# Attention stage of a fused kernel: k's turns and copy ahead of y's, squares behind, a second mask that waits for the decay, an earlier signal for constants

## The reference

```python
B, H, S, D = q.shape                       # 4, 8, 768, 48
f = 1.0 / (1.0 + np.exp(-f_logit))
for t in range(S):
    state = f[:, :, t, :, None] * state + np.einsum('bhd,bhe->bhde', k[:, :, t], v[:, :, t])
    y[:, :, t] = np.einsum('bhd,bhde->bhe', q[:, :, t], state)
```

```python
h = np.maximum(x[mask] @ w1[e], 0.0)
out[mask] = gate_w[mask, None] * (h @ w2[e])
```

## Time and profile before

| | us |
|---|---|
| median of three runs | 681.18 |
| lowest, highest | 680.19, 682.83 |
| the profiled execution: whole | 683.31 |
| the profiled execution: span of the trace | 681.5 |
| TensorE busy in the span | 627.3 (92%) |
| VectorE busy | 442.8 (65%) |
| ScalarE busy | 310.7 (46%) |
| GpSimd busy | 171.2 (25%) |
| mean granted clock of TensorE | 0.969 of full speed |

### The profile page before, as it was taken

How to read it: one execution, slowest core, us unless ns; L and a number is a source line. 1 busy time by engine, 2 the same in 40 slices (tenths; PEclk the granted TensorE clock), 3 DMA queues, 4 the chain that set the end, 5 groups by cost and what they waited for, 6 DMA issues and landing times.

```text
span 681.5 us, 15527 instructions
## 1 busy us (share of the span) xinstructions
PE 627.3 (92%) x4935; PEld 587.0 (86%) x4936; DVE 442.8 (65%) x964; ACT 310.7 (46%) x519; POOL 171.2 (25%) x200
## 2 busy tenths in 40 slices
PE   4999999999639999999999999995799999999997
PEld 3778788787539999999999999894799999999997
DVE  5878998989745674948383756645267446547752
ACT  2566757766404344534343344341356336336640
POOL 7212226263440005041313224052110110110111
PEclk9999999999959999999999999997799999999999
DMA  9997887772143452718070736421385474474610
GB/s 152 138 187 154 200 128 173 109 165 47 46 151 116 160 188 102 260 34 272 23 261 32 269 103 209 164 90 63 98 281 161 145 260 133 148 254 141 235 36 24
DMA packets 144217, 100.68 MB, mean 148 GB/s; under 512 B 106319, under 2 KB 135098, under 8 KB 144176
## 3 DMA queue, kind: packets, MB, share of 16 engines
q1 hardware_dynamic: 137008, 87.42, 47.8%
q0 software_dynamic: 7168, 12.73, 5.2%
HBM read 79.46 MB, written 30.08 MB: 161 GB/s over the span
## 4 chain that ended last, share of the span: by engine, by line
PE 76%; DVE 10%; issue 6%; ACT 4%; POOL 2%; SPq 1%; DMA 0%; DVEq 0%; ACTq 0%; POOLq 0%
PE bank_a L963 7%; PE bank_a L965 7%; PE bank_a L964 7%; PE banks_y L974 3%; PE banks_y L973 3%; PE banks_y L972 3%; PE bank_b L963 3%; PE banks_s L811 2%; PE bank_b L965 2%; PE bank_b L964 2%; PE banks_s L985 2%; PE bank_b L761 2%; PE bank_b L973 2%; PE bank_b L974 2%; PE bank_b L972 2%
## 5 line engine op out<-in xcount | busy, mean ns | idle before, releaser
L1371 DVE TENSOR_TENSOR w_lo<-raw_w,w_hi 128x768 fp32r<-128x768 f32 x128 | 115.0, 951 | 34.1 <-ACT w_hi L1105 34.0
L1105 ACT ACTIVATE w_hi<-raw_w 128x768 fp32r<-128x768 f32 x128 | 99.1, 836 | 10.3 <-issue 10.3
L963 PE MATMUL bank_a<-x_hi,w_hi 128*128 128x384 f32 (+2 forms) x288 | 97.8, 340 | 1.3 <-DVE x_lo L1718 0.7
L964 PE MATMUL bank_a<-x_lo,w_hi 128*128 128x384 f32 (+2 forms) x288 | 95.3, 331 | 0.0
L965 PE MATMUL bank_a<-x_hi,w_lo 128*128 128x384 f32 (+2 forms) x288 | 95.3, 331 | 0.0
L666 POOL DMA_INDIRECT sorted_rows<-row_send,slot_idx x32 | 34.0, 1062 | 202.7 <-DVE slot_idx L1707 195.4
L676 POOL DMA_INDIRECT out<-row_send,out_idx x24 | 24.2, 1008 | 174.3 <-DVE row_send L1774 157.1
L963 PEld LDWEIGHTS bank_a<-x_hi,w_hi 128*128 128x128 f32 x288 | 54.2, 188 | 6.2 <-issue 4.2
L965 PEld LDWEIGHTS bank_a<-x_hi,w_lo 128*128 128x128 f32 x288 | 54.1, 188 | 0.9
L1293 ACT ACTIVATE h_hi<-bank_a 128x384 fp32r<-128x384 f32 (+1 forms) x48 | 21.6, 450 | 72.9 <-PE bank_a L965 72.8
L964 PEld LDWEIGHTS bank_a<-x_lo,w_hi 128*128 128x128 f32 x288 | 54.1, 188 | 0.8
(11 more groups left out here) (275 smaller groups left out, 1543.1 us busy)
## 6 DMA issues: line engine op xcount, KB each, us to landing
raw_w<-in_moe_w SPq DMA_DIRECT2D x30, 1536.0 KB
sorted_rows<-pad_row SPq DMA_DIRECT2D x8, 582.0 KB
raw_f<-in_f_logit SPq DMA_DIRECT2D x32, 144.0 KB
raw_k<-in_k SPq DMA_DIRECT2D x32, 144.0 KB, 3.2
raw_q<-in_q SPq DMA_DIRECT2D x32, 144.0 KB, 3.8
raw_v<-in_v SPq DMA_DIRECT2D x32, 144.0 KB, 3.4
xs<-sorted_rows SPq DMA_DIRECT2D x11, 388.0 KB, 3.2
xs<-sorted_rows SPq DMA_DIRECT2D x19, 194.0 KB, 3.0
```

Of the source, the lines that this page charges most:

```text
L963: pe.matmul(bank, hi, x_hi[:, kd, 0:size], start=(kd == 0), stop=False)
L964: pe.matmul(bank, hi, x_lo[:, kd, 0:size], start=False, stop=False)
L1105: act.activation(w_hi[:, sl, :], raw_w[:, sl, :], ACT.Copy).then_inc(w_split_hi, 1)
L1371: dve.tensor_tensor(w_lo[:, sl, :], raw_w[:, sl, :], w_hi[:, sl, :].bitcast(F32), ALU.subtract).then_inc(w_split_lo, 1)
```

## The change

- GpSimd fills cols and counts const_ready right behind the fills of rows, ahead of twelve other fills and copies.
- TensorE: k's turns become turn_k(g). It is called once before the loop and then in pair_tail, for the next pair, after turn_pair and before from_scores of the second half. In pair_head the wait for y_copied moves behind the first scores, and so do the rank products; in the last pair turn_pair moves behind u. The second half's copied scores are waited for in every pair.
- ScalarE: the copy of k_rows becomes copy_k(g), called once before the loop and then ahead of the copy of y. The square of pair g - 2 stands at the head of pair g, behind the copy of y, no more behind copy_rows.
- GpSimd's mask of the second half waits for decay of the next pair, which VectorE now counts (decay_ready).
- VectorE: add_logits comes ahead of route_norm, and logit_sum has two buffers, by batch.
- The embedding's turns go to a part of bank_s[1] of their own (ps_emb), in the tail of pair 1 instead of its head, and their copies on ScalarE behind the second half's scores.

```diff
+        ps_emb = bank_s[1][:, 384:384 + (KD + HP) * E]
...
+            pool.memset(cols[:], 0.0).then_inc(const_ready, 1)
             ch.link(pool.memset(pad_row[:], 0.0))
...
-            pool.memset(cols[:], 0.0).then_inc(const_ready, 1)
...
                 pool.wait_ge(score_copied, 2 * g + half + 1)
+                if half == 1 and g + 1 < PAIRS:
+                    pool.wait_ge(decay_ready, g + 2)
...
+            def turn_k(g):
+
+                pe.wait_ge(kup_ready, g + 1)
+                pe.wait_ge(exp_ready, min(g + 2, PAIRS))
+                for c in range(C - 1):
+                    ins = pe.transpose(bank_s[c // 4][:, (c % 4) * P:(c % 4 + 1) * P], k_up[g % 2][:, c * P:(c + 1) * P], ident[:])
+                ins.then_inc(krow_ready, 1)
+
             def pair_head(b, hp, last):
...
-                pe.wait_ge(kup_ready, g + 1)
-                pe.wait_ge(exp_ready, g + (1 if last else 2))
-                for c in range(C - 1):
-                    ins = pe.transpose(bank_s[c // 4][:, (c % 4) * P:(c % 4 + 1) * P], k_up[par][:, c * P:(c + 1) * P], ident[:])
-                ins.then_inc(krow_ready, 1)
                 if not last:
...
-                pe.wait_ge(y_copied, g + 1)
-                if g == 1:
-                    emb_transpose()
-                if last:
-                    turn_pair(g - 1)
-                if hp == 3 and b > 0:
-                    rank(gs[0], b + 1, C, ps_rank, ps_count)
                 pe.wait_ge(qdown_ready, g + 1)
                 pe.wait_ge(krow_copied, g + 1)
                 score_half(g, par, 0)
+                pe.wait_ge(y_copied, g + 1)
+                if hp == 3 and b > 0:
+                    rank(gs[0], b + 1, C, ps_rank, ps_count)
...
                 else:
+                    turn_pair(g - 1)
...
                     turn_pair(g - 1)
+                if not last:
+                    turn_k(g + 1)
                 pe.wait_ge(score_masked, 2 * g + 2)
                 from_scores(par, 1).then_inc(y_ready, 1)
...
+            def copy_k(g):
+
+                act.wait_ge(krow_ready, g + 1)
+                if g > 0:
+                    act.wait_ge(u_ready, g)
+                act.activation(k_rows[:].rearrange("p c x -> p (c x)"), banks_s[:, 0:(C - 1) * P], ACT.Copy).then_inc(krow_copied, 1)
...
-                act.wait_ge(krow_ready, g + 1)
-                act.activation(k_rows[:].rearrange("p c x -> p (c x)"), banks_s[:, 0:(C - 1) * P], ACT.Copy).then_inc(krow_copied, 1)
+                if g > 1:
+                    square(g - 2)
                 copy_scores(g, 0)
...
                     copy_rows(g - 1)
-                    square(g - 1)
...
+                if not last:
+                    copy_k(g + 1)
                 act.wait_ge(y_ready, g + 1)
...
-                ch.link(dve.scalar_tensor_tensor(out=decay[:], in0=guess_error[:], scalar=2.0, in1=decay_guess[:],
-                                                 op0=ALU.add, op1=ALU.mult))
+                dve.scalar_tensor_tensor(out=decay[:], in0=guess_error[:], scalar=2.0, in1=decay_guess[:],
+                                         op0=ALU.add, op1=ALU.mult).then_inc(decay_ready, 1)
+                dve.wait_ge(decay_ready, g + 1)
...
+                if g > 0:
+                    add_logits(ch, g - 1)
                 if hp == 1 and b > 0:
                     route_norm(ch, b - 1, gs[0])
-                    ch.link(dve.tensor_tensor(logit[:], logit_sum[:], bc(norm[:, 7, :], C), ALU.mult))
-                if g > 0:
-                    add_logits(ch, g - 1)
+                    ch.link(dve.tensor_tensor(logit[:], logit_sum[(b - 1) % 2][:], bc(norm[:, 7, :], C), ALU.mult))
```

More of the change, by code:

```diff
@@ L115, in gla_moe_program @@
         logit = sb("logit", [P, C, E])
-        logit_sum = sb("logit_sum", [P, C, E])
+        logit_sum = [sb(f"logit_sum{i}", [P, C, E]) for i in range(2)]
         sq_pairs = sb("sq_pairs", [P, C, HP])
@@ L223, in gla_moe_program @@
         log_ready = sem("log_ready")
-        kup_ready, qdown_ready = sem("kup_ready"), sem("qdown_ready")
+        kup_ready, qdown_ready, decay_ready = sem("kup_ready"), sem("qdown_ready"), sem("decay_ready")
         krow_ready, krow_copied = sem("krow_ready"), sem("krow_copied")
@@ L838, in pair_tail @@
                 pe.wait_ge(score_copied, 2 * g + 1)
+                if g == 1:
+                    emb_transpose()
                 score_half(g, par, 1)
                 pe.wait_ge(state_ready, g + 1)
-                if g == 1:
-                    pe.wait_ge(emb_t_copied, 1)
                 from_state(par)
@@ L845, in pair_tail @@
                 from_scores(par, 0)
+                pe.wait_ge(score_copied, 2 * g + 2)
                 if f_next:
-                    pe.wait_ge(score_copied, 2 * g + 2)
+                    if g == 1:
+                        pe.wait_ge(emb_t_copied, 1)
                     pe.wait_ge(f_in[par], 32 * ((HP // 2) * b + hp // 2 + 2))
@@ L902, in _ @@
                     pe.matmul(bank[:, c * P:(c + 1) * P], zeros[:], zeros[:], start=True, stop=True)
+            turn_k(0)
             for g in range(PAIRS):
@@ L1156, in pair_tail @@
                 copy_scores(g, 1)
+                if g == 1:
+                    act.wait_ge(emb_t_ready, 1)
+                    act.activation(emb_t[:].rearrange("p k e -> p (k e)"), ps_emb[:, 0:KD * E], ACT.Copy)
+                    act.activation(pair_turn[:, :, 2 * D:PAIR_TURN], ps_emb[:, KD * E:(KD + HP) * E].rearrange("p (k e) -> p k e", k=HP),
+                                   ACT.Copy).then_inc(emb_t_copied, 1)
                 if hp == 1 and b > 0:
@@ L1434, in add_logits @@
                 dve.wait_ge(rows_copied, g + 1)
-                total, part = logit_sum[:].rearrange("p (a c) e -> p a c e", a=2), ps_turned[:, :, :, 2 * D:PAIR_TURN]
+                total, part = logit_sum[g // HP % 2][:].rearrange("p (a c) e -> p a c e", a=2), ps_turned[:, :, :, 2 * D:PAIR_TURN]
                 if g % HP == 0:
@@ L1531, in _ @@
             add_logits(ch, PAIRS - 1)
-            ch.link(dve.tensor_tensor(logit[:], logit_sum[:], bc(norm[:, 7, :], C), ALU.mult))
+            ch.link(dve.tensor_tensor(logit[:], logit_sum[(B - 1) % 2][:], bc(norm[:, 7, :], C), ALU.mult))
             pick(ch, gs[0], B - 1)
```

12 lines of the change are left out of this document (4 added, 8 removed).

## The result

The changed kernel takes **672.36 us** (median of 4, 671.59 to 672.50); the kernel before, timed again beside it, 680.68 (4 runs, 679.87 to 682.83). The ratio is 0.9871, with a 95% interval from 0.9846 to 0.9895: 1.3% faster. The forecast was 675.5, with a range from 672.5 to 679.6.

A forecast was written before the change was run, and what follows sets the result against it. TensorE was taken to bound an ordinary pair, with one wait on ScalarE and VectorE close behind. Start -2.5, pairs -3.8 and end +0.6 gave -5.7 us: 675.5 from the median 681.18, range 672.5 to 679.6.

The forecast's parts named there:

- The ordinary pair: Attention stage, pairs without routing work: TensorE's 0.76 us wait for k_rows goes, so 10.43 us becomes 9.67.
- the pair of the norm total: Fourth pair of the first batch, with the norm total but no row sends: 9.82 us.
- the five slacks: Ordinary pair: k_rows free by 0.6 us, y's copy 0.7, logit_sum about 0.2, state 0.35, and the second mask's wait hidden.
- the narrow one: ScalarE in an ordinary pair: squares behind y's copy end at 3.0, scores' copy due at 3.1, cover 0.1 us wide.
- The routing pairs: Four pairs of each later batch: 11.16 us with a 1.49 state stall behind route_norm's 1.84, then 10.57, 9.67 and 10.2.
- The rule weighed: VectorE and GpSimd lock shared SBUF ports per instruction, so scans lose nothing; even sharing would add 0.5 us, forecast 677.0.
- The start: Up to T of g = 1: earlier cols signal gains 2.5 us; 1 if loads land late, 3.5 if they don't matter.
- The end: Last pairs: mask stall and turn_pair(14) ahead of score_half delay the last sum_squares by 0.6 us, between 0 and 1.5.
- VectorE gives back more: Rival: scans lose to masks, sends cost fully, masks come later; up to 4.3 us lost, 677 to 680; chance 0.27.
- More is gained: Rival: no stalls at mask or sends, lossless end, start of -3.4; up to 3.5 us more, half 673; chance 0.13.
- Slower: Rival: the mask's wait for decay delays y's chain in all nine routed pairs, 1.1 us each; 685; chance 0.08.
- The wait only moves: Rival: the next wait (y, state or logit_sum's bank) takes k's gain back, start lost among loads; 681; chance 0.05.

The follow-up runs named there:

- route_first: The changed kernel with route_norm and logit ahead of add_logits again, both logit_sum buffers kept: 668.52 us, ratio 0.9841 to the kernel before.
- after_moved_back: The changed kernel plus an unused 64-byte tile, putting load rows 96 bytes behind a multiple of 256 as before: 677.33 us, ratio 0.9904.
- before_again: The kernel before, without an edit, run for a second profile: 684.27 us, ratio 1.0000.
- early_cols_only: The kernel before with only the fill of cols and its signal moved early: 683.33 us, ratio 0.9988.
- after_at_160: The changed kernel plus an unused 128-byte tile, so load rows start 160 bytes behind a multiple of 256: 674.16 us, ratio 0.9904.
- after_again: The changed kernel once more, without an edit: 671.88 us, ratio 0.9884 to the kernel before.
- late_cols: The changed kernel with the fill of cols and its signal back at the end of GpSimd's list: 675.62 us, ratio 0.9943.
- early_cols_moved: The kernel before with the early fill of cols and an unused 192-byte tile that moves the loads' addresses: 682.49 us, ratio 0.9984.
- before_moved: The kernel before with only an unused 192-byte tile, giving later tiles their addresses of the changed kernel: 684.46 us, ratio 1.0004.
- k_order_only: The changed kernel with route_norm ahead of add_logits, without the second mask's wait for decay and without the early cols signal: 678.92 us, ratio 0.9918.

## Why the prediction came out as it did

**The ordinary pair** was right: 9.60 us against 9.67, the pair of the norm total 9.89 against 9.82 (0.21 of it for state), and the five slacks held, the narrow one too.

**The routing pairs.** I forecast 11.16, 10.57, 9.67 and 10.2 us; they took 10.77, 10.48, 9.60 and 10.23. This is where the larger part of the miss lies. The stall for state was there, 1.10 instead of 1.49. The term that was mis-sized is the 1.84 us of route_norm, which I took over from the earlier trace rows. There its second instruction takes 0.45 us because GpSimd's copy of carry runs beside it, as in route_first:

```profile
71.51 0.45 DVE L1335 TENSOR_TENSOR norm<-norm 128x6 f32<-128x6 f32 x1
```

```profile
71.34 0.59 POOL L632 COPY carry<-decay 128x240 f32<-128x240 f32 x1
```

Behind add_logits it runs alone and takes 0.17, and the whole 1.56 (72.56 to 74.12). That gives 0.28 of the 0.39; the state products were also due 0.12 later than I had them, which makes the stall shorter. The waits for the mask, 0.41 against 0.45, and behind the row sends, 0.55 us each, were as forecast. The pairs gained 4.93 instead of 3.8: 0.8 from the two route_norm pairs, 0.2 from the pairs behind them, the rest from the ordinary ones.

**The rule weighed** held. The mask that met a scan in the route_norm pair took 1.78 us and the scan kept its 1.76. That is what the Trainium skill, "SBUF — State Buffer", section "SBUF: two separate sides", says of the exclusive lock. Even sharing, which would have cost 0.5 in each such pair, is refuted by that row.

**The start** is where the reasoning failed, and not only a size. I carried -2.5 and measured -3.25 from T of g = 1 (35.90 to 32.65). The sentence that was wrong is that the second logit_sum buffer costs nothing by itself: it moves the loads' tiles off the crossing. With the old addresses, in after_moved_back, the start gains 2.2 us (34.48 to 32.27) where I had 2.5, and the load of pair 1 ends at 15.4, as I had it; the addresses give the other 0.9. The two profiles of the kernel before start 0.3 apart (34.48 and 34.17 in before_again), so these sums hold to about that. One time in the chain was wrong as well: the logarithm for pair 1 could not start at 18.0 when its scan was put at 18.26. The scan moved too, and the logarithm ran at 17.66. I had also not read the granted clock there. In the kernel before it is 0.50 while the first turns of k_rows and of raw k run, behind the wait for cols:

```profile
16.00:18.00 2.00, 2.00 (x11) 1.81 (x9) 1.93 (x3) 0.71 (x1) 0.00 (x0) 0.50 1.50 179
```

In the changed kernel it is 1.00 in that stretch, and so it is in after_moved_back. It is 0.50 in early_cols_only and in after_at_160, where TensorE waits some 1.5 us for the load. The low clock by itself need not cost anything: after_again has 0.50 from 14 to 16 us, behind a wait of 1.90 us, and its first scores take 1.65 us, yet it starts at 31.31, like the first trace. There the longer rows lie in the time that TensorE otherwise waits for q_down (0.46) and for state (0.48):

```profile
14.51 1.65 PE L814 MATMUL banks_s<-q_down,k_up 64*128 64x128 f32 x12
```

The same early signal is worth 0.2 us where the slow loads take its place, with their wait and the low clock behind it (early_cols_only), and 3.4 where they don't (late_cols against after_again, early_cols_moved against before_moved). What the clock adds can be estimated from the list of work that takes 5.35 us in after_moved_back: it takes 6.73 in early_cols_only (15.38 to 22.11), 6.47 in late_cols and 6.95 in before_moved, so 1.1 to 1.6 us in each. Of the 1.9 us by which early_cols_only starts behind early_cols_moved, 1.4 is the clock by this estimate, and 0.5 is left for the later end of the load.

**The end** was right within 0.1: from T of g = 13, as I had counted it, 0.7 us longer (23.38 to 24.07) against 0.6.

**The sum.** The stage ends 7.5 us earlier instead of 5.7: 0.75 of the difference is the start, 1.1 the pairs, and the end takes 0.1 back. So two steps failed. The cost of the second logit_sum buffer was put at nothing, and its addresses gave 0.9 of the start. The 1.84 us of route_norm was carried over from an order in which a GpSimd copy ran beside it, and measured 1.56. The medians differ by 8.3, and the interval of the ratio reaches from 7.1 to 10.5 us of gain, so nothing beyond the stage is needed. The profiled executions differ by 10.9; that of before had the long handover, 11.7 us against 6.6, and of these 5.0 us 2.0 had come back by the end of the span, for a reason that the views read here don't show.

**The rivals.** *VectorE gives back more* fell: no scan lost to a mask, and the sends cost 0.55. *More is gained* lay nearest, by the wrong means. All its 3.5 us give 672.0, and half of them 673.7 (not 673 as I wrote), with 672.36 between the two. But of its four parts only the larger gain of the start came, while the mask, the sends and the end cost what the forecast said. *Slower* fell: its condition was met in the three pairs named, at 0.41, 0.41 and 1.03 us, and leaving the wait out changed nothing. *The wait only moves* fell in the ordinary pairs and holds in the route_norm pairs alone, where the new wait for state, 1.10 us, is more than the old one for k_rows, 0.76 at most. The range ended at 672.5, above the 672.0 that this rival gives in full, and it held no case in which a buffer's address matters.

## What to carry to other kernels

Put work of an engine ahead of a wait, not behind it: route_norm ahead of the wait for rows_copied is worth 3.4 us here, and with it the mask's wait for decay gains 1.9 us in the pairs, against 0.5 without. Look at where tiles lie in SBUF when a change adds a buffer, and keep short rows that a load writes from crossing a multiple of 256 bytes; it costs time where a wait for loads is on the path, as at the start here. And measure a part both alone and left out: early_cols_only (0.2 us) and late_cols (3.4 us) together showed that something else was in play.

## What the runs showed of the hardware

- Loads that write rows of 192 bytes fill the queue at 163 to 164 GB/s when most rows cross a multiple of 256 bytes in SBUF, and at 201 to 238 when those of f, k and q do not; they land after 4.4 to 4.7 us against 2.8 to 3.3. Rows that start at 96 and at 160 are equally slow, and those that start at 0, 32 and 64 equally quick within the spread of the runs. No row of another length was run.
- Between 12 and 20 us TensorE's granted clock was at the lower level (0.50 in at least one stretch of 2 us, or 0.53 to 0.60) behind waits of 1.53 to 4.6 us: in before, before_again, before_moved, early_cols_only, k_order_only, after_again and after_at_160. The length of the wait alone doesn't decide it. Behind 1.55 us at 25.5 in early_cols_moved it stayed at 1.00, and in route_first six turns took 1.49 us behind a wait of 0.85.
- The profile's granted clock can miss it: in late_cols, in route_first and in the first turns of every trace (4 to 9 us) six turns take 1.49 to 1.54 us instead of 0.88 where it says 1.00. The lengths of the rows were the surer sign.
- What half the clock costs depends on the waits behind it: 1.5 us of start in after_at_160 against after_moved_back, nothing in after_again.
- From SyncE's last issue of pad_row to its first row load of the second expert stage it took 11.6 to 11.7 us in all eight kernels of two sessions and 6.6 to 7.7 in all seven of the other two, with and without the change, on one chip both. The first profile of before, 11.7 beside 6.6 in that of the changed kernel, shows that it can also differ between two profiles taken apart.
